# The third expert's weights reloaded among the gathers, the first expert's low parts on VectorE, and twelve probability copies on ScalarE

## What is computed

```python
# 1. attention, causal, window of 64
scores = where(0 <= i - j < 64, q @ k.T / 8, -1e9)
x = (softmax(scores) @ v) as [2304, 512]
# 2. mixture of 8 experts, the best two for each token
noisy = x @ w_gate + log1p(exp(x @ w_noise)) * noise
top2 = two largest of noisy; share = softmax of the two
for each expert e and its tokens:
    out[mask] += share * (relu(x[mask] @ w1[e]) @ w2[e])      # w1: 512x1024, w2: 1024x512
# 3. dense layer with a smooth ramp
h = out @ w_in                                                # 512x2048
g = h if h >= 1, 0 if h <= -1, else (h + 1)**2 / 4
return g @ w_out                                              # 2048x512
```

## Time and profile before

| | |
|---|---|
| median of 3 runs | 1081.92 us |
| the profiled execution's own time | 1086.34 us |
| its span, first to last instruction | 1084.7 us |
| mean granted TensorE clock | 0.995 |
| share of the chain that ended last | PE 81%, DVE 5%, DMA 4%, POOL 3%, issue 3%, ACT 1% |
| attention loop | about 9 to 120 us |
| routing to the first tile | about 120 to 149 us |
| 42 expert tiles | about 149 to 675 us |
| dense layer | about 675 to 1084.7 us |

### The profile page before, as it was taken

How to read it: one execution, slowest core, us unless ns; L and a number is a source line. 1 busy time by engine, 2 the same in 40 slices (tenths; PEclk the granted TensorE clock), 3 DMA queues, 4 the chain that set the end, 5 groups by cost and what they waited for, 6 DMA issues and landing times.

```text
span 1084.7 us, 17735 instructions
## 1 busy us (share of the span) xinstructions
PE 1058.8 (98%) x5848; PEld 883.2 (81%) x5849; DVE 350.6 (32%) x696; ACT 350.4 (32%) x809; POOL 411.8 (38%) x327
## 2 busy tenths in 40 slices
PE   8999979998999999999999999999999999999998
PEld 6988758886888888888888887988888888888886
DVE  6889741121122111221122212333332233333222
ACT  5557432122222222222222221523334334335333
POOL 6226578558755527081370905940010001100000
PEclk9999999998999999999999999999999999999999
DMA  7675645995442414233142322240011102101001
GB/s 200 202 225 173 219 139 192 318 327 206 155 155 95 156 39 146 91 130 116 41 176 65 125 98 68 79 136 20 20 39 48 31 1 79 39 1 39 1 1 39
DMA packets 50195, 120.09 MB, mean 111 GB/s; under 512 B 7072, under 2 KB 12320, under 8 KB 49632
## 3 DMA queue, kind: packets, MB, share of 16 engines
q0 software_dynamic: 16688, 62.66, 17.6%
q1 hardware_dynamic: 19920, 32.62, 9.8%
q10 hardware_dynamic: 13536, 24.12, 6.5%
HBM read 86.88 MB, written 32.51 MB: 110 GB/s over the span
## 4 chain that ended last, share of the span: by engine, by line
PE 81%; DVE 5%; DMA 4%; POOL 3%; issue 3%; ACT 1%; SPq 1%; another core or an unknown queue 1%; POOLq 0%; ACTq 0%; DVEq 0%
PE bank L1538 6%; PE bank L1540 6%; PE bank L1539 6%; PE bank L1473 6%; PE bank L1492 6%; PE bank L1490 6%; PE bank L1491 6%; PE bank L1475 6%; PE bank L1474 6%; PE bank L1531 6%; PE bank L1532 6%; PE bank L1533 6%; PE bank L1498 3%; DMA x_sorted<-gath_a 2%; POOL Wl L479 2%
## 5 line engine op out<-in xcount | busy, mean ns | idle before, releaser
L479 POOL TENSOR_TENSOR Wl<-stage,Wh 128x2048 fp32r<-128x2048 f32 x36 | 165.7, 4604 | 3.0
L1140 DVE COPY y_out<-bank 128x512 f32<-128x512 f32 x42 | 29.1, 692 | 358.8 <-PE bank L1492 351.1
L1473 PE MATMUL bank<-Wh,xT_h 128*128 x336 | 136.3, 406 | 6.3 <-POOL Wl L479 4.9
L1178 DVE SCALAR_TENSOR_TENSOR bank<-bank,square 128x512 f32<-128x512 f32 x72 | 50.4, 700 | 254.9 <-ACT square L829 254.9
L1475 PE MATMUL bank<-Wh,xT_l 128*128 x336 | 132.3, 394 | 0.0
L1474 PE MATMUL bank<-Wl,xT_h 128*128 x336 | 131.7, 392 | 0.0
L1492 PE MATMUL bank<-Wh,hT_l 128*128 x336 | 131.0, 390 | 0.0
L1490 PE MATMUL bank<-Wh,hT_h 128*128 x336 | 130.8, 389 | 0.1
L1491 PE MATMUL bank<-Wl,hT_h 128*128 x336 | 130.8, 389 | 0.0
L800 ACT ACTIVATE hT_h<-bank 128x512 fp32r<-128x512 f32 x84 | 45.7, 596 | 248.0 <-PE bank L1498 245.3
L477 POOL CAST Wh<-stage 128x2048 fp32r<-128x2048 f32 x36 | 68.5, 1904 | 148.0 <-PE bank L1492 144.4
(11 more groups left out here) (236 smaller groups left out, 1753.0 us busy)
## 6 DMA issues: line engine op xcount, KB each, us to landing
stage<-w POOLq DMA_DIRECT2D x32, 1024.0 KB
y_sorted<-y_out ACTq DMA_DIRECT2D x42, 256.0 KB
x_in<-x_sorted ACTq DMA_DIRECT2D x38, 256.0 KB
x_sorted<-gath_b SPq DMA_DIRECT2D x20, 256.0 KB
v_ring<-vW SPq DMA_DIRECT2D x36, 128.0 KB, 4.9
x_rows<-x_blk SPq DMA_DIRECT2D x36, 128.0 KB, 3.2
x_sorted<-gath_a SPq DMA_DIRECT2D x18, 256.0 KB
k_ring<-kT SPq DMA_DIRECT2D x8, 512.0 KB, 5.5
```

Of the source, the lines that this page charges most:

```text
L479: nc.gpsimd.tensor_tensor(Wl[:, s, cols], stage[:, c % 2], Wh[:, s, cols], ALU.subtract).then_inc(w_ready, 1)
L1473: nc.tensor.matmul(H_ps[a][:], xT_h[:, u, k], high, start=(k == 0), stop=False)
```

## The change

1. GpSimd does `reload(2, 2, 0)` and `fetch_first(3)` ahead of gather 24, behind a wait for `tables_ready`. `reload(3, 3, 1)` and `fetch_first(4)` then stand first behind the last gather, and the loop begins one pair later.
2. `low_piece` moves from GpSimd to VectorE: piece k at the end of VectorE's step 25 + k, pieces 14 and 15 ahead of routing. ScalarE casts piece k in step 24 + k, one earlier. GpSimd asks for the first two quarters at spread 23, for the third behind spread 33, for the fourth and the second expert's first two behind the last spread, each after its `w_ready`.
3. The expert's number is read once for a pair of transfers, not once for each.
4. In twelve steps (15, 16, 17, 19 to 23, 26, 29, 32, 35) ScalarE copies `probsT` ahead of its exponentials, and VectorE doesn't.
5. TensorE does no `early_hidden` in step 37; in step 40 it does the first four of the 24, and 20 instead of 18 behind.

```diff
+BY_SCALAR = (15, 16, 17, 19, 20, 21, 22, 23, 26, 29, 32, 35)
...
+            def expert_at(m):
+                return None if isinstance(m, str) else pool.value_load(order[0:1, bass.ds(m, 1)], min_val=0, max_val=E - 1)
-            def raw(m, c):
+            def raw(m, c, expert):
...
-                expert = pool.value_load(order[0:1, bass.ds(m, 1)], min_val=0, max_val=E - 1)
...
-            def load_raw(m, c, after=None):
-                if after:
-                    pool.wait_ge(*after)
-                src, k = raw(m, c)
+            def load_raw(m, c, expert):
+                src, k = raw(m, c, expert)
                 pool.dma_start(stage[:, c % 2].rearrange("p (k n) -> p k n", k=k), src).then_inc(staged[c % 2], 16)
...
-            def low_piece(k):
-                c, cols = k // PIECES, slice(PC * (k % PIECES), PC * (k % PIECES) + PC)
-                pool.wait_ge(piece_cast, k + 1)
-                inst = nc.gpsimd.tensor_tensor(Wl[:, 0, PC * k:PC * k + PC], stage[:, c % 2, cols],
-                                               Wh[:, 0, PC * k:PC * k + PC], ALU.subtract)
-                if k % PIECES == PIECES - 1:
-                    inst.then_inc(w_ready, 1)
-                    load_raw(c // 2, (c + 2) % 4, (w_ready, c + 1))
+            def load_raw_when(m, c, count):
+                expert = expert_at(m)
+                pool.wait_ge(w_ready, count)
+                load_raw(m, c, expert)
...
             for s in range(8, G):
                 spread(s)
-                if s == 24:
+                if s == 23:
                     pool.wait_ge(order_ready, 1)
-                    load_raw(0, 0)
-                elif s == 25:
-                    load_raw(0, 1)
+                    fetch_first(0)
                 elif s == 29:
                     early_gather()
-                if s >= 30:
-                    low_piece(s - 30)
-            for k in range(G - 30, 4 * PIECES):
-                low_piece(k)
+                if s == 33:
+                    load_raw_when(0, 2, 1)
+            load_raw_when(0, 3, 2)
+            load_raw_when(1, 0, 3)
+            load_raw_when(1, 1, 4)
...
+                if t == 3 * GB:
+                    pool.wait_ge(tables_ready, 1)
+                    reload(2, 2, 0)
+                    fetch_first(3)
                 if GB <= t < GB + DIRECT:
                     pool.wait_ge(xg_done, t - GB + 1)
...
-            pool.wait_ge(tables_ready, 1)
-            with pool.Fori(1, E // 2 - 1) as m:
+            reload(3, 3, 1)
+            fetch_first(4)
+            with pool.Fori(2, E // 2 - 1) as m:
...
+                if s in BY_SCALAR:
+                    act.wait_ge(pT_done, s - 1)
+                    act.wait_ge(pv_done, s - 2)
+                    nc.scalar.activation(probsT[:], PT_ps[:], ACT.Copy).then_inc(pT_copied, 1)
...
-                if s >= 25:
-                    cast_piece(s - 25)
+                if s >= 24:
+                    cast_piece(s - 24)
...
+            def low_piece(k):
+                c, cols = k // PIECES, slice(PC * (k % PIECES), PC * (k % PIECES) + PC)
+                dve.wait_ge(piece_cast, k + 1)
+                inst = nc.vector.tensor_tensor(Wl[:, 0, PC * k:PC * k + PC], stage[:, c % 2, cols],
+                                               Wh[:, 0, PC * k:PC * k + PC], ALU.subtract)
+                if k % PIECES == PIECES - 1:
+                    inst.then_inc(w_ready, 1)
...
-                if 2 <= s < G + 2:
+                if 2 <= s < G + 2 and s not in BY_SCALAR:
                     dve.wait_ge(pT_done, s - 1)
...
                 early_step(s)
+                if s >= 25:
+                    low_piece(s - 25)
...
             nc.vector.memset(picked[:, NT], 0.0).then_inc(zeroed, 1)
+            for k in range(G + 3 - 25, 4 * PIECES):
+                low_piece(k)
...
-                if s == G + 1:
+                if s == G + 4:
                     pe.wait_ge(w_ready, 2)
                     pe.wait_ge(exl_ready, 1)
                     pe.wait_ge(exp_done, G - 1)
-                    early_hidden(0, 2)
-                if s == G + 4:
-                    early_hidden(2, 6)
+                    early_hidden(0, 4)
...
-            early_hidden(6, 24)
+            early_hidden(4, 24)
```

More of the change, by code:

```diff
@@ L460, in hold, with fetch_first @@
                 pool.sem_inc(passed, 1)
-            def load_raw(m, c, after=None):
-                if after:
-                    pool.wait_ge(*after)
-                src, k = raw(m, c)
+            def load_raw(m, c, expert):
+                src, k = raw(m, c, expert)
                 pool.dma_start(stage[:, c % 2].rearrange("p (k n) -> p k n", k=k), src).then_inc(staged[c % 2], 16)
-            def fetch_first(m, pace=(None,) * 2):
+            def fetch_first(m):
+                expert = expert_at(m)
                 for c in range(2):
-                    load_raw(m, c, pace[c])
+                    load_raw(m, c, expert)
             def parts(n, s, c):
@@ L486, in first_parts @@
                     hold(w_ready, 4 * n + c + 1)
-                    load_raw(m, c + 2)
+                    load_raw(m, c + 2, expert)
             def last_parts(n, s):
@@ L622, in _, with reload @@
                 pool.wait_ge(x_stored[r], 32 * (NT // CH))
+            def reload(m, n, s):
+                used = pool.value_load(last_tile[0:1, bass.ds(n - 2, 1)], min_val=1, max_val=TILES + 1)
+                hold(y_done, used)
+                first_parts(m, n, s)
+                last_parts(n, s)
             for t in range(TILES):
@@ L741, in _ @@
                 step(s)
-            for k in range(G + 4 - 25, 4 * PIECES):
+            for k in range(G + 4 - 24, 4 * PIECES):
                 cast_piece(k)
```

## The result

The changed kernel takes 1077.55 us (median of six executions, 1076.53 to 1078.33). The kernel before, run beside it, takes 1082.63. The ratio is 0.9943 with a 95% interval of 0.9926 to 0.9959. So the change is faster, by about 5 us, where 11.1 had been forecast. On a second chip it was 1077.37 against 1083.97, 6.6 us.

The account below looks back on a forecast made before the run. TensorE, busy 98% of the span, was taken as the bound, so only its waits could give time back. The terms -7.6 - 2.15 - 0.85 - 0.5 made -11.1 us, from 1081.9 to 1070.8, range 1068.0 to 1075.0.

Parts of the forecast that it names:

- Part 1: Tile 9: with the third expert's reload among the gathers, TensorE's wait and the clock fall go, -7.6 us.
- the 226.4 of the working: Time in us at which tile 9's first half would be ready, 30 us before it is wanted.
- -7.6: Tile 9's loss in one trace, 19.84 less 12.24 us, 4.87 of it wait, taken as won in full.
- the same difference: Whole kernel: the median lies 4.4 us below the profiled execution, before and after the change alike.
- Rival (c): Tile 9: gathers faster in unprofiled runs, stall smaller, only about 4 us won there; 1074.5 us, chance 0.07.
- Part 2: Attention loop: probability copies on ScalarE relieve VectorE and end the first two losses, -2.15 us.
- costs at most the copy, and a step and a half lies between them and their reader: Attention loop: ScalarE has room for the copies, 0.65 us each, ahead of its exponentials.
- Part 3: Steps 25 to 35: low parts on VectorE win 1.15 us less 0.3 of new waits, -0.85 us.
- the lower end of the bound: Steps 25 to 35: new waits between 0 and 2.0 us, 0.3 taken.
- rival (a): Steps 25 to 40: VectorE becomes the bound and costs 2 to 3 us; about 1073.5 us, chance 0.12.
- The third quarter's transfer: Weights' third part, needed one step earlier, keeps a budget near 10 us; cost nothing.
- Part 4: Tail and routing: tail 0, bounds -0.5 and +1.2 us; L1050 falls from 0.82 to about 0.31, -0.5 us.

Follow-up runs that it names:

- experiment 1: Kernel before with only the third expert's reload and the fetch behind it moved ahead of gather 24: 1081.13 us, ratio 0.9971.
- experiment 6: Kernel before with only the expert's number read once for a pair of transfers: 1081.21 us, ratio 0.9981.
- experiment 2: Changed kernel without the moved reload, the single read of the expert's number kept: 1078.66 us, ratio 0.9952.
- experiment 3: Changed kernel with ScalarE's probsT copies only in steps 16, 18, 20, 22, 26, 28, 32, 34: 1077.34 us, ratio 0.9934.
- guard: Changed kernel plus six matmuls that nobody reads, put ahead of the scores of step 4: 1077.53 us, ratio 0.994.

## Why the prediction was wrong

**Part 1, the reload: mechanism right, size wrong.** The reload came behind gather 23, as said; the wait at tile 9 went and the clock stayed at 1.00. The second low part ended at 218.96 + 4.62 = 223.6, and tile 9's first half was ready sooner than the 226.4 of the working. The gathers went on at 241.21 (forecast near 245), the fourth reload began at 272.30 (forecast near 280), and tile 14 shows no wait. In that trace the term was 7.59 where 7.60 had been forecast. The step that failed is the next one: that the difference of one trace holds for the median. The stall of before is 4.2 us in the mean of four traces, and 3.1 us is what experiment 1 measured for the move alone. The failed term is -7.6, in whose place stands about -4: 3.4 of the 6.7 us by which the forecast missed.

There was a hint in what was known: the profiled execution took 1086.3 us where the other runs had 1080.7 to 1082.5. The working took "the same difference" of 4.4 us from the forecast, as if it were a cost of being profiled that both kernels share. The changed kernel's profiled execution took 1077.91 with a median of 1077.55, so it isn't. It belonged to the executions of before, and the stall was the place in the trace that could hold it. Rival (c) said just this, and gave 1074.5; it had a chance of 0.07 and was the one that came. Only its reason was off: a profiled execution of before can be as quick as any, as the second trace with 1081.9 us shows. What differs is the execution. It still lies 3 us below the measured time. Of these 1.2 us are the loop's (part 2 below), and 0.7 are the starting value: the median of before was 1081.92 in three executions and is 1082.63 in six, and 1083.7 to 1084.2 on the other chips. The last 1.1 us no run splits further.

**Overlooked: the single read.** The diff's change of `load_raw` was not costed: the prediction has no term for it. It shortens the same stall (experiment 6), so it adds nothing to the sum of the whole change, but it changes who earned it: by the traces most of the stall goes with the read alone (one trace each: 1.02 us of wait left in experiment 6 and 0.57 in experiment 2, where the four traces of before have 3.3 in the mean).

**Part 2, the copies: half given back.** The pairs' delays went, as said. The step that failed is that the wait of the exponentials behind the copy "costs at most the copy, and a step and a half lies between them and their reader". The exponentials' reader was not what came late. Behind them in ScalarE's own queue stands its copy of the transposed x, and TensorE reads that with its next instructions. ScalarE's timeline in step 35 shows the order (the fourth of each kind of instruction is left out):

```profile
111.66 0.60 ACT L711 ACTIVATE probsT<-bank 128x512 f32<-128x512 f32 x1 [0.95 <-PE bank L1310]
112.15 0.36 ACT L717 ACTIVATE probs<-bank,bias 128x128 f32<-128x128 f32 x1
...
113.52 0.62 ACT L726 ACTIVATE xT_blk<-bank 128x512 f32<-128x512 f32 x1
```

and TensorE's, what it costs:

```profile
114.28 0.41 PE L1320 MATMUL bank<-ident,x_blk 128*128 128x128 f32 x2 [0.64 <-ACT xT_blk L726]
```

The kernels of experiment 3, which have no copies in odd steps, get back 0.76 us of the loop. For the whole attention loop the forecast was -3.0, the change has -1.8 (mean of two traces against four), and the even steps reach -2.35 (mean of four against the same four).

**Part 3, the low parts: right.** No wait of TensorE names VectorE between 27 and 110 us, and the small instructions are hardly stretched any more (the former L1008 of the earlier trace rows, its longest was 1218 ns):

```profile
L1025 DVE TENSOR_SCALAR rowsum_g<-rowsum x36: 156/160/399, 14.2 to 118.7; 128x4 f32<-128x4 f32 x36
...
L906 DVE TENSOR_TENSOR Wl<-stage,Wh x16: 681/682/815, 83.8 to 121.2; 128x512 fp32r<-128x512 f32 x16
```

Of the sixteen pieces the longest takes 815 ns, 0.13 us above the median. So the value near the lower end of the bound was the right one, and rival (a) did not come. By the rule of the Trainium skill (SBUF — State Buffer, SBUF: two separate sides) these pieces contend with GpSimd's q_bd copies, and the one that comes second waits.

The trace agrees, but most of the waiting is on GpSimd's side. Four groups of four copies, from 82.5 to 100.1 us, have a piece beside them; this is the third:

```profile
93.73 2.11 POOL L530 COPY q_bd<-q_ring 64x256 f32<-64x256 f32 x4 [2.92 <-issue]
```

They take 2.06 to 2.21 us, where four copies with no piece beside them take 1.76 to 1.80 in this trace. In each group the one copy that starts while a piece runs takes 0.69 to 0.84 us and not 0.40, and ends 0.26 or 0.27 us behind the piece. The one long piece starts while a copy runs. The price in time is nothing that shows: in these steps no wait of TensorE names GpSimd. The third quarter's transfer, costed at nothing, was nothing: no wait of ScalarE names it.

**Part 4, tail and routing: right.** L1071, the former L1050, takes 0.31 us, not the 0.82 of the earlier trace rows:

```profile
123.34 0.31 DVE L1071 TENSOR_TENSOR t_a<-noisy,rest 128x144 f32<-128x144 f32 x1 [0.82 <-ACT rest L757]
```

From step 35 to the first gather it is 0.5 us less, as said. (The tail has two waits of its own now, 0.64 as above and 0.49 for a copy of VectorE; they don't show in that sum.)

**The start: not in the prediction at all.** TensorE waits for GpSimd's q_bd in the first steps for a time that differs by execution, and the clock may fall behind it. After, in stretches of 2 us (columns as above):

```profile
14.00:16.00 2.00, 0.46 (x4) 0.44 (x5) 0.98 (x4) 0.90 (x6) 1.18 (x3) 1.00 1.06 204
16.00:18.00 2.00, 2.00 (x20) 1.67 (x20) 0.97 (x2) 0.10 (x1) 1.66 (x6) 0.68 1.02 324
18.00:20.00 2.00, 2.00 (x20) 1.73 (x17) 1.14 (x4) 1.41 (x8) 1.68 (x6) 0.50 1.04 408
```

Step 8 starts at 25.64 in the first trace of before, the earliest of all traces here, and at 26.9 to 31.0 in five others of kernels with the old loop (three of before, and experiments 1 and 6); at 27.0 to 28.2 in five with the new loop and no guard. The means are 27.8 and 27.6: the change has no part in it. So the trace that the prediction rested on had the worst tile 9 and the best start, and the start hid part of what was unusual in it.

**The sum again, from traces that repeat.** Mean of four traces of before against two of after: tile 9 -4.2, loop -1.8, route -0.5, first gather to tile 8 -0.5 (this stretch varies by 0.5 us in the four traces of before and by 0.9 in the two of after), start +1.15, rest +0.1: -5.7 us of span. Without the start, which is chance, -6.9. The medians say -5.1 and -6.6. Nothing of size is missing.

What stays open: why the gathers' idle times differ from execution to execution; how much of the unprofiled executions' spread (1078.3 to 1089.5 for the kernel before) is tile 9 and how much the start, since only profiled executions have rows; and whether the guard is worth its place.

**The best version** is the changed kernel with the copies in the eight even steps and the guard: 1075.71 and 1076.67 us on two chips, 0.9924 and 0.9937 of the kernel before. The change as it was given had 0.9943 and 0.9938, so by these intervals it can't be called better.

## What to carry to other kernels

Here a stall behind a queue with DMA waits in it had another length in each execution. Before a term of one trace is put into a sum, ask whether the profiled execution lies apart from the median. If so, suspect the largest such stall, do not carry the difference over to both kernels, and take a second trace. An engine's copy that is moved to another engine delays what stands behind it there; follow that queue to the first instruction that TensorE reads, which need not be the next one. And a register load in front of each transfer is work on a queue that is late: read it once.

## What the runs showed of the hardware

- Waits at one place had two prices. At tile 9, after 3.64 and 3.39 us without work TensorE's granted clock was 1.00 in the stretch behind, and the loss was the wait and 0.2 to 0.3 us. After 4.87 us it was 0.50 (the 1.2 GHz level), and the loss was the wait and 2.7 us. At the start it fell after much less: to 0.68 and 0.50 after a wait of 2.05 us, some 4 us behind one of 0.42, while in the third trace of before it stayed at 1.00 behind waits of 1.31 and 1.34 us.
- Reading the expert's number anew between a low part and the transfer behind it costs GpSimd 0.6 to 1.2 us of idle time (1.34 to 1.99 against 0.76), though no instruction in the profile shows it.
- The gathers' time is fixed only as long as nothing holds them. An undisturbed one follows the last after 1.26 us, and up to gather 12 four traces of one kernel agree to 0.01 us. Behind it single idle times for a bounce reach 4.7 us and differ from trace to trace, and from the first gather to the third expert's reload it is 99.9 to 102.7 us.
- A VectorE subtraction with two inputs in SBUF and a GpSimd copy in SBUF slow each other: GpSimd's 64x256 copies took 0.69 to 0.84 us beside one, 0.40 alone.
